# Attention in a new order on every engine, with GpSimd's port waits, 640-byte stores and an early loop

## What is computed

```python
for t in range(S):                                   # S = 768, per batch and head; D = 40
    y[:, :, t] = einsum('bhd,bhde->bhe', rt, state)
    Sa = einsum('bhde,bhe->bhd', state, at)
    state = state * wt[:, :, None, :] - einsum('bhd,bhe->bhde', Sa, bt) + einsum('bhd,bhe->bhde', vt, kt)
x = y as (B, S, H * D)
u = x + real(fft2(x));  x = u + relu(norm(u) @ w_ch1) @ w_ch2
u = x + (relu(x.T @ w_tok1) @ w_tok2).T;  out = u + relu(u @ w_ch1') @ w_ch2'
```

## Time and profile before

| | us |
|---|---|
| median of 3 runs (lowest, highest) | 1118.55 (1118.51, 1119.64) |
| profiled execution | 1119.17 |
| its span | 1117.2 |
| busy: TensorE, VectorE, ScalarE, GpSimd | 989.0, 555.2, 339.3, 272.7 |

### The profile page before, as it was taken

How to read it: one execution, slowest core, us unless ns; L and a number is a source line. 1 busy time by engine, 2 the same in 40 slices (tenths; PEclk the granted TensorE clock), 3 DMA queues, 4 the chain that set the end, 5 groups by cost and what they waited for, 6 DMA issues and landing times. The chain is left out here.

```text
span 1117.2 us, 47338 instructions
## 1 busy us (share of the span) xinstructions
PE 989.0 (89%) x20860; PEld 931.4 (83%) x20861; DVE 555.2 (50%) x943; ACT 339.3 (30%) x740; POOL 272.7 (24%) x239
## 2 busy tenths in 40 slices
PE   6777888888888874789699999999889999999996
PEld 3667778887777874678599999999889999999996
DVE  3435677766776633865744444444863332223330
ACT  1334454554544532223222222222222221112220
POOL 4434554555545520640140000000800000000000
PEclk9778999999999985889899999999989999999998
DMA  7333665555665525520110000000400000000000
GB/s 226 98 100 101 188 190 173 163 161 171 190 188 160 162 78 158 155 89 0 42 41 1 0 0 0 0 0 4 126 0 1 18 18 18 14 4 18 18 18 18
DMA packets 68715, 86.85 MB, mean 78 GB/s; under 512 B 30578, under 2 KB 48242, under 8 KB 68658
## 3 DMA queue, kind: packets, MB, share of 16 engines
q1 hardware_dynamic: 67842, 82.52, 24.5%
q0 software_dynamic: 816, 3.60, 1.1%
HBM read 70.37 MB, written 7.86 MB: 70 GB/s over the span
## 5 line engine op out<-in xcount | busy, mean ns | idle before, releaser
L1236 ACT ACTIVATE d_h_hi<-d_bank 128x384 fp32r<-128x384 f32 x96 | 47.2, 492 | 197.7 <-PE d_bank L1341 197.7
L1296 DVE SCALAR_TENSOR_TENSOR d_h_lo<-d_bank,d_h_hi 128x384 fp32r<-128x384 f32 x96 | 53.6, 558 | 76.0 <-ACT d_h_hi L1236 76.0
L1355 PE MATMUL d_bank<-w_hi,d_h_lo 128*128 128x320 f32 x288 | 89.0, 309 | 0.0
L1355 PE MATMUL d_bank<-w_hi,d_h_hi 128*128 128x320 f32 x288 | 89.0, 309 | 0.0
L1355 PE MATMUL d_bank<-w_lo,d_h_hi 128*128 128x320 f32 x288 | 88.9, 309 | 0.0
L1236 ACT ACTIVATE c_h_hi<-c_bank 128x384 fp32r<-128x384 f32 x80 | 37.6, 490 | 142.8 <-PE c_bank L1341 142.8
L1355 PE MATMUL c_bank<-w_hi,c_h_hi 128*128 128x320 f32 x240 | 74.8, 312 | 0.0
L1355 PE MATMUL c_bank<-w_hi,c_h_lo 128*128 128x320 f32 x240 | 74.1, 309 | 0.0
L1355 PE MATMUL c_bank<-w_lo,c_h_hi 128*128 128x320 f32 x240 | 74.1, 309 | 0.0
L787 POOL CAST w_hi<-stage 128x1280 fp32r<-128x1280 f32 (+2 forms) x13 | 15.0, 1155 | 215.8 <-DMA stage<-in_moe_w_ch 215.8
L1308 DVE TENSOR_TENSOR d_o<-d_bank,u_all 128x320 f32<-128x320 f32 x24 | 11.8, 492 | 111.0 <-PE d_bank L1355 111.0
(11 more groups left out here) (212 smaller groups left out, 2805.8 us busy)
## 6 DMA issues: line engine op xcount, KB each, us to landing
e_raw<-in_e SPq DMA_DIRECT2D x72, 256.0 KB, 6.1
r_raw<-in_c SPq DMA_DIRECT2D x24, 768.0 KB, 4.3
tok<-tok_of SPq DMA_DIRECT2D x24, 320.0 KB, 6.6
e_raw<-in_e SPq DMA_DIRECT2D x24, 260.5 KB, 5.7
va<-in_c SPq DMA_DIRECT2D x24, 160.0 KB, 3.9
vb<-in_c SPq DMA_DIRECT2D x24, 160.0 KB, 4.2
attention_out<-yout SPq DMA_DIRECT2D x96, 40.0 KB, 5.0
stage<-in_moe_w_ch POOLq DMA_DIRECT2D x4, 640.0 KB, 6.1
```

Of the source, the lines that this page charges most:

```text
L1236: nc.scalar.activation(h_hi[:, m, :], bank[m % 4][:, 0:TW], ACT.Relu).then_inc(h_hi_done, 1)
L1296: nc.vector.scalar_tensor_tensor(h_lo[:, m, :], bank[m % 4][:, 0:TW], 0.0, h_hi[:, m, :].bitcast(F32), ALU.max, ALU.subtract).then_inc(h_l ...
L1355: last = nc.tensor.matmul(bank[4 + t % 2][:, 0:E], lhs, rhs, start=(m == 0 and i == 0), stop=(m == NM - 1 and i == 2))
```

## The change

- All five orders are new. TensorE's window now begins with `sol0` and ends with `abk`. Offsets are deeper: `rv`, `ru`, `y_s`, `y_k`, `upd_k`, `upd_b` at -3 (were -2), the doubling steps at -1, `tokb`, `tokk`, `tokd` at -1 (were 0). SyncE's window is `e`, `va`, `cp`, `vb`, `rr`, `store`. PSUM banks are assigned anew.
- `PORT_AFTER`: on GpSimd `at` of group n also waits for `xs` of n - 1, `nt0` for `suff` of n + 1, `mt0` for `decay` of n + 1.
- Heads are paired as (q a), in the packing of the inputs (on the host) and in `xv`, so that a partition's four heads are one run of 640 bytes in DRAM.
- TensorE writes out only window 0, in which only `abk` has a group, after 8 idle products; its loop runs window 1 to 23. Steps whose group doesn't exist yet run in the loop on cleared tiles; `EMPTY` says how many times. For them the other engines release `ready` with writes of one element (`empty`), TensorE counts up the DMAs' ones, and waits on `filled` count the empty groups in (`passed`, `EXTRA`). Windows 24 to 26 stay straight. More tiles are cleared first (six memsets on GpSimd, eleven copies on ScalarE), and the constants are loaded from ScalarE's queue and not SyncE's. The waits at n = 0, n = 1 or in the last group go or move accordingly.

The diff, cut: where steps only change place among TensorE's units, and where a wait guarded by `if n >= 1` becomes `passed`, one case stands for all.

```diff
-ORDER_SP = [("store", -5), ("vb", -4), ("va", -2), ("rr", -3), ("e", 0), ("cp", -3)]
-ORDER_DVE = [("decay", -1), ("m1", -2), ("y", -4), ("u", -3), ("xs", -2), ("m2", -2), ("n8", -2), ("suff", 0), ("aa", -1), ("ak", -1),
-             ("rv", -3), ("xt", -3), ("ru", -3), ("du2", -2)]
-ORDER_POOL = [("t_neg", -2), ("kt", -1), ("at", -1), ("nt0", -1), ("bt", 0), ("xs2", -1), ("mt0", -1)]
-ORDER_PE = [("n4", -1), ("m1", -1), ("res3", -2), ("y_b", -3), ("n4t", -1), ("sol3", -2), ("xsd", -2), ("m2", -1), ("rhs_v", -1),
-            ("n8", -1), ("rhs_a", -1), ("ut", -2), ("m3", -1), ("tokb", 0), ("abk", 0), ("sol0", -1), ("tokk", 0), ("res1", -1),
-            ("rv", -2), ("upd_k", -2), ("sol1", -1), ("upd_b", -2), ("nn0", 0), ("ru", -2), ("res2", -1), ("n2", 0), ("n2t", 0),
-            ("y_s", -2), ("sol2", -1), ("tokd", 0), ("y_k", -2)]
-ORDER_ACT = [("res2", -2), ("n2", -1), ("n2t", -1), ("n4", -1), ("res3", -2), ("n4t", -1), ("tokd", -1), ("xsd", -2), ("rhs", -1),
-             ("m3", -1), ("ut", -2), ("du0", -1), ("tokb", 0), ("tokk", 0), ("res1", -1), ("du1", -1), ("nn0", 0)]
+ORDER_SP = [("e", 0), ("va", -1), ("cp", -3), ("vb", -3), ("rr", -2), ("store", -4)]
+ORDER_DVE = [("xt", -4), ("u", -3), ("xs", -2), ("y", -4), ("m2", -2), ("n8", -2), ("suff", 0), ("aa", -1), ("ak", -1), ("decay", 0),
+             ("rv", -3), ("ru", -3), ("du2", -2), ("m1", -1)]
+ORDER_POOL = [("at", -1), ("nt0", -1), ("mt0", -1), ("bt", 0), ("kt", 0), ("t_neg", -1), ("xs2", -1)]
+ORDER_PE = [("sol0", -2), ("tokb", -1), ("tokd", -1), ("res1", -2), ("tokk", -1), ("rv", -3), ("sol1", -2), ("nn0", -1), ("ru", -3),
+            ("res2", -2), ("n2", -1), ("y_s", -3), ("sol2", -2), ("n2t", -1), ("y_k", -3), ("m1", -1), ("res3", -2), ("upd_k", -3),
+            ("upd_b", -3), ("n4", -1), ("sol3", -2), ("xsd", -2), ("y_b", -3), ("n4t", -1), ("rhs_v", -1), ("m2", -1), ("rhs_a", -1),
+            ("n8", -1), ("ut", -2), ("m3", -1), ("abk", 0)]
+ORDER_ACT = [("nn0", -1), ("res2", -2), ("n2", -1), ("n2t", -1), ("res3", -2), ("n4", -1), ("xsd", -2), ("n4t", -1), ("rhs", -1),
+             ("m3", -1), ("ut", -2), ("du0", -1), ("tokb", 0), ("tokd", 0), ("res1", -1), ("tokk", 0), ("du1", -1)]
+
+BANKS = {"abk": (True, 0), "upd_k": (True, 1), "y_s": (True, 0), "ru": (True, 1), "rv": (True, 0), "tokd": (True, 1), "m3": (True, 1), "nn0": (False, 0), "n2": (False, 0), "n2t": (False, 1), "m1": (False, 0), "n4": (False, 0), "n4t": (False, 0), "m2": (False, 1), "n8": (False, 0), "xsd": (False, 1), "ut": (False, 1), "tokb": (False, 0), "tokk": (False, 1), "y_k": (True, 0), "y_b": (True, 0), "upd_b": (True, 1)}
+PORT_AFTER = {"at": ("xs", -1), "nt0": ("suff", 1), "mt0": ("decay", 1)}
+EMPTY = {"m3": 1, "du0": 1, "r": 2, "res1": 1, "du1": 1, "rv": 2, "res2": 1, "cp": 2, "du2": 1, "vb": 2, "res3": 1, "u": 1, "xsd": 1}
+WARM = {"abk": 8}
+FIRST = 1
+EXTRA = {name: max(0, -ahead - FIRST) for name, ahead in ORDER_PE}
-WARM = {"abk": 44, "nn0": 10, "n2": 5}
...
-    def windows(order, run):
-        for g in range(-max(a for _, a in order), NG - min(a for _, a in order)):
+    def windows(order, run, empty=None):
+        for g in range(-max(EMPTY.values()), NG - min(a for _, a in order)):
             for name, ahead in order:
                 if 0 <= g + ahead < NG:
                     run(name, g + ahead)
+                elif empty and g + ahead < 0 and g + ahead + EMPTY.get(name, 0) >= 0:
+                    empty(name)
+
+    def passed(eng, name, groups):
+        if groups + EXTRA[name] > 0:
+            eng.wait_ge(filled[name], groups + EXTRA[name])
...
-    xv = x_dram.rearrange("b (i t) (a q e) -> b i q t a e", t=C, a=HA, q=2)
+    xv = x_dram.rearrange("b (i t) (q f) -> b i q t f", t=C, q=2)
...
-                if n >= 1:
-                    sp.wait_ge(filled["rv"], n)
-                    sp.wait_ge(filled["ru"], n)
-                    sp.wait_ge(filled["y_k"], n)
+                passed(sp, "rv", n)
+                passed(sp, "ru", n)
+                passed(sp, "y_k", n)
...
-                        sp.dma_start(xv[2 * bp + b, i, par], yout[n % 2][tok_half(par ^ b), b, :, :]).then_inc(stored[n % 2], 16)
+                        sp.dma_start(xv[2 * bp + b, i, par], yout[n % 2][tok_half(par ^ b), b, :, :].rearrange("p a d -> p (a d)")).then_inc(stored[n % 2], 16)
...
+        for x in (t_neg, rv_t, ru_t, minv, rhs_b, res_b):
+            nc.gpsimd.memset(x[:, :, :], 0.0).then_inc(rest_cleared, 1)
+        gp.wait_ge(consts_in, 64)
+        nc.gpsimd.tensor_copy(eye_b[:, :], eye[:, :]).then_inc(eye_done, 1)
+        unused = iter(range(32))
+
+        def empty(name):
+            k = next(unused)
+            nc.gpsimd.memset(spare[0][0:1, k:k + 1], 0.0).then_inc(ready[name], 1)
...
+            if name in PORT_AFTER:
+                x, later = PORT_AFTER[name]
+                if 0 <= n + later < NG:
+                    gp.wait_ge(done[x], n + later + 1)
...
+        for dst, src in ((eye[:, :], "eye"), (ident[:, :], "ident"), (block[:, :], "block"), (masks[:, :, :].rearrange("p i c -> p (i c)"), "masks")):
+            act.dma_start(dst, consts[src]).then_inc(consts_in, 16)
+        act.wait_ge(cleared, CLEARED)
...
+        for x in ("va", "vb", "r", "cp"):
+            if x in EMPTY:
+                pe.sem_inc(ready[x], amount(x) * EMPTY[x])
...
+        for g in range(FIRST):
             for name, ahead in ORDER_PE:
-                if 0 <= g + ahead:
-                    if g + ahead == 0:
-                        keep_busy(WARM.get(name, 0))
+                if g + ahead >= 0:
+                    keep_busy(WARM.get(name, 0))
                     unit(name, g + ahead)
-        with pe.Fori(first, NG):
+        pe.wait_ge(rest_cleared, REST_CLEARED)
+        with pe.Fori(FIRST, NG):
             for name, ahead in ORDER_PE:
                 unit(name)
-        for g in range(NG, NG + first):
...
```

More of the change, by code:

```diff
@@ L335, in _, with empty @@
             nc.vector.memset(x[:, :], 0.0).then_inc(cleared, 1)
+        unused = iter(range(32))
+        def empty(name):
+            k = next(unused)
+            nc.vector.memset(spare[1][0:1, k:k + 1], 0.0).then_inc(ready[name], 1)
         def run(name, n):
@@ L595, in unit @@
                 last.then_inc(filled["res1"], 1)
+            if name == "tokk":
+                for a in range(HA):
+                    last = nc.tensor.transpose(out[:, a * P:a * P + P], kt[:, 2 * a:2 * a + 2, :].rearrange("p q t -> p (q t)"), ident[:, :])
+                last.then_inc(filled["tokk"], 1)
             if name == "rv":
+                if n == NG - 1:
+                    pe.wait_ge(done["y"], NG - 1)
+                take(n, "ak", 2)
                 take(n, "r")
@@ L665, in unit @@
                 last.then_inc(filled["n2"], 1)
[L666 to L670 removed]
             if name == "y_s":
[L672 removed]
+                take(n, "rv")
                 for a, b, par in every:
@@ new lines, in unit @@
+            if name == "res3":
+                take(n, "du2")
+                for a, b, par in every:
+                    q, j = tok_half(par), 2 * a + b
+                    last = mm(pr[tok_half(par ^ b), b, a * D:a * D + D], t_neg[q, j, :], du[2][q, j, :], False, True)
+                    took(n, 4 * a + 2 * b + par, last, "du2")
+                last.then_inc(filled["res3"], 1)
+            if name == "upd_k":
+                if n == NG - 1:
+                    pe.wait_ge(ready["ru"], NG)
+                take(n, "vb")
+                for a, b, par in every:
+                    q, j = tok_half(par), 2 * a + b
+                    last = mm(out[own(b), par, a * D:a * D + D], tok[q, 1, j, :], vb[q, j, :], a == 0, False)
+                    took(n, 4 * a + 2 * b + par, last, "vb")
+                last.then_inc(filled["upd_k"], 1)
@@ new lines, in unit @@
+            if name == "upd_b":
+                for a, b, par in every:
+                    q, j = tok_half(par), 2 * a + b
+                    last = mm(out[own(b), par, a * D:a * D + D], tok[q, 0, j, :], u[q, j, 0:D], False, True)
+                last.then_inc(filled["upd_b"], 1)
+            if name == "n4":
+                take(n, "n2t")
+                take(n, "m1")
+                for j, par in halves:
+                    q = tok_half(par)
+                    last = mm(out[q, j * C:j * C + C], nt[1][q, j, :], nn[1][q, j, :])
+                    took(n, 2 * j + par, last, "n2t", "m1")
+                last.then_inc(filled["n4"], 1)
@@ new lines, in unit @@
+            if name == "sol3":
+                take(n, "res3")
+                for a, b, par in every:
+                    q, j, c = tok_half(par ^ b), 2 * a + b, (1 * HA + a) * D
+                    last = mm(pr[tok_half(par), b, c:c + D], minv[q, j, :], res_b[q, j, :], False, True)
+                    took(n, 4 * a + 2 * b + par, last, "res3")
+                last.then_inc(filled["sol3"], 1)
+            if name == "xsd":
+                for a in range(HA):
```

(59 more changed lines are left out.)

372 lines of the change are left out of this document (111 added, 261 removed).

## The result

The changed kernel takes 1084.82 us (median; 1084.45 to 1086.13), the kernel before 1119.1 beside it: a ratio of 0.9693 with a 95% interval of 0.9676 to 0.9710, about 34 us less. The profiled execution of after has a span of 1083.4 us at a mean granted clock of 0.963, against 1117.2 and 0.952. The forecast was 1076 (1058 to 1100): the direction and the range held, and 9 us of the saving did not come.

A forecast was written before the change was run, and what follows sets the result against it. Only attention could move: TensorE's passes of 15.40 us, some 3.8 of it waits and handovers, plus start and end. 1119.2 - 21 (steady passes) - 23 (start) + 1 (end) = 1076.2, less 0.6: 1076 us, range 1058 to 1100.

The forecast's parts named there:

- 8 us for fetch and cold clock: Start of attention: 8 us added to the first passes for fetching code and the colder clock, giving group 4 at 79.
- Rival B: Start: empty groups' small writes queue behind real work, the first pass starves, the start gives only 7; 1092 us, chance 0.13.
- The walk: Steady pass: TensorE's new order timed unit by unit from `abk` at 0, giving 13.76 us before additions.
- the loop's end: Steady pass: 0.27 us added for the gap where TensorE's loop branches back.
- 0.25 for handovers: Steady pass: 0.25 us added for TensorE's handovers between kinds of unit.
- Rival A: Steady pass: stays at 15.4 us because the two chains slip against the walk; 1097 us, chance 0.15.
- one clause on it: Steady pass: the `vb` wait, 10.8 us in 19 passes, goes, as `upd_k` moves to two thirds of the pass.
- rival C: SyncE's order starves VectorE: slow stores, landing and `suff` make a pass 16.65 us; 1121 us, chance 0.06.
- The 1.6 us for four stores: SyncE: issuing a group's four stores in 640-byte runs takes 0.4 us each, against 3.10 us for four before.
- The chain: `aa`, `nn0`, `y_k`, `r_raw`, stores, landing of `e`, `suff`, `aa` again: 13.2 us, or 14.2 with slower landing; no cost.
- Port waits at 0: GpSimd: the three waits of `at`, `nt0` and `mt0` for VectorE are met or lie in slack, costing 0.
- the +1: Tail of attention: straight code of 53 units instead of 36 takes 42 us against 41.0, +1 (-3 to +6).

The follow-up runs named there:

- the single swap: The kernel before with the load of `vb` ahead of the four stores in SyncE's window, nothing else: 1102.21 us, ratio 0.9843.
- The run with 42.85 us for the same code: The changed kernel with TensorE's windows 1 and 2 written out straight and the loop from window 3 on: 1103.01 us, ratio 0.9857.

## Why the prediction came out as it did

**The start: direction right, size 4.7 us too large.** The prediction put `abk` of group 0 at 13.9 and group 4 at 79; they came at 14.63 and 83.5. The late first group is 0.7: `at` ends only at 14.5. The six memsets did not delay it; GpSimd is through with them at 5.7, waits 2.2 us for the constants and then for its load, and `kt` takes 0.97 us longer beside `suff` of group 1. The prediction costed collisions of the two engines in the steady pass and none here. The passes cost 4 x 0.27 = 1.1 more than the 14.3 assumed. The term that was mis-sized is "8 us for fetch and cold clock": it measured 83.5 - 14.63 - 4 x 14.57 = 10.6, of which the first pass has 8.2, the second 1.1, and a fall of the clock in the fourth 1.2. I had put all of it into the first pass, and for that pass alone 8 was right: 5.7 of slower products and 2.5 of stops. The reading of the stops as the cost of code met for the first time held: two windows written straight cost 15.0 us by group 4. The Trainium skill's rule on unrolling ("Runtime: NRT & Kernel Launch", Instruction fetch mechanics) would have had the loop give nothing here. The run with two straight windows says otherwise, with TensorE standing up to 2.27 us at a time in them and 3.75 in the loop's first pass; the branch back costs 0.27 us, as read before. Rival B is refuted, and what gave it a chance too, the small writes of the empty groups: between 14 and 84 us the waits of TensorE for other engines are 2.9 us for `at`, 2.5 for `m2` and 0.9 for `n8`, the same as in later passes, and none for these writes.

**The steady pass: 14.57 undisturbed, 14.63 on average, instead of 14.3.** The walk was followed to the unit: relative to `abk`, `sol0` came at 1.19 (walk 0.93), `tokd` at 2.05 (1.63), `y_k` at 6.88 (6.22), `m2` at 11.04 (10.21), `rhs_a` at 12.29 (11.50), the next `abk` at 14.57 (13.76). The lag grows to 0.83 by `m2` and no further. Of it 0.27 is the loop's end, as said. The other 0.56 is the term "0.25 for handovers", the one that was mis-sized: behind each full transpose TensorE stands 0.17 us ("issue" at 203.32 and 211.12), so a transpose costs 0.59 from start to next start and not 0.42, and three lie ahead of `m2`, 0.5 of the 0.56. Against the 14.3 that is 0.27 us a pass, 5.1 us in all; one pass in which the granted clock was 0.89 (15.82 by `at`) is another 1.2. Both stalls that the walk left, at `rhs_a` and at `abk`, are where it left them. Rival A is refuted.

**`vb`: right place, too little weight.** The prediction wrote one clause on it. It was the main thing: the single swap gives nearly the same pass as the whole change, 14.69 on average against 14.63. With it, the kernel before stands 1.07 us at `rhs_a` for `m2`, then waits for `at`, and needs 14.50; the changed kernel has the same two waits and needs 14.57. That was there to be read: the walk of the new order ends in the same stall of 1.04 us as the earlier trace rows, so what it took out elsewhere could not shorten that part, and I should have asked what the old order gives without its `vb` wait.

**The stores and rival C.** The 1.6 us for four stores was wrong, 2.38 was measured; I had taken the 0.33 of `r_raw`'s issue for an effect of long rows, and the run with short ones shows 0.13 of it. `e` landed after 4.79 (211.75 to 216.54), not 4.4. The chain came to 14.3 us and not 13.2, inside the pass by a few tenths, so C did not decide, but it was nearer than its 0.06 says: as soon as the pass fell to 14.14 it showed, as 18.4 us of waits. Two of the signs of being wrong that the prediction names, `suff` waiting over 1 us for `e_raw` and `aa` for `suff`, are in the changed kernel's own trace (1.30 us and 0.6 in the pass shown) without setting its pass.

**Port waits at 0** was right, to 0.04 us a pass. **The end** came 2.6 us better than the +1, with stops of 1.74, 0.94, 1.25 and 2.13 us in the straight windows; how much of them lay beside other waits was not worked out. The run with 42.85 us for the same code shows how little a forecast of such stops is worth, so this error, which helped the total, was luck. Attention's last `yout` came at 400.4 and not near 393.

The errors add up to the difference: 4.7 + 6.4 - 2.6 + 0.7 = 9.2, against 1084.8 - 1076 = 8.8.

## What to carry to other kernels

- Where an engine waits for a DMA, read what stands ahead of that DMA in the issuing engine's queue before reordering anything else; one exchange may be all. A recorded wait does not say what its removal gives: 10.8 us of waits for `vb` gave 13.3, and 18.4 us of `suff`'s waits gave 1.9.
- Where a chain through two engines has a fixed length (`m2`, then `rhs_a` and `at`), put units of other groups into its gaps; that, with the stores ahead of `r_raw`, gave 20 us more than the change did.
- Code that an engine meets for the first time costs more than its operations. Enter the loop as early as cleared tiles allow, and don't pay for a warm clock with more products than it saves.
